# Attention in groups of two tiles: the order of one fused kernel changed

## The chip, the cores and the metric

The kernel runs on one core of a Trainium2 chip. A core has TensorE (matmuls), VectorE, ScalarE, GpSimd and SyncE, each with an instruction queue of its own; they meet only in semaphores. The metric is the device time of one execution in microseconds.

## What is computed

Three layers in a row, all in float32, for 2 batches of 768 positions and 512 channels:

```python
# 1. attention, 2 x 8 heads of 64: sinks (first 4 keys) and a window of 128 keys
keep = is_sink | ((rel >= 0) & (rel < window))
a = softmax(where(keep, q @ k.T / sqrt(64), -1e9));  x = a @ v      # heads side by side: [2, 768, 512]
# 2. mixing of positions
theta = x @ w_theta;  y = w_tok_r @ (x * cos(theta)) + w_tok_i @ (x * sin(theta))
u = x + y;  x = u + relu(u @ w_ch)
# 3. gated layer
h = relu(x @ w_in);  u, v = halves(h);  v = layer_norm(v)
out = (u * (w_spatial @ v + b_spatial)) @ w_out
```

The change touches attention and the first products with w_theta.

## The kernel before

A **pair** is two heads of one batch; there are eight pairs (n = 0..3, batch b = 0, 1, no = 2n + b), each of six **tiles** of 128 queries, 48 tiles m in all. A tile needs the keys of its own 128 positions, of the 128 before and of the sinks. Two heads stand in the two halves of the partitions.

What each engine does for tile m (i = m mod 6):

- **scores** (TensorE, L1079): six matmuls, three products of high and low parts for each head, and a bias of two small matmuls, into one of two banks s_ps. It waits until the exps of tile m-2 have read that bank.
- **maxima** (VectorE, L787): L793 folds the two key blocks into one, where the mask chooses, then one L799 for each head takes the maximum. Tile 0 of a pair needs no fold.
- **exps** (ScalarE, L521): one exp for each head, and its sum, into probs.
- **turn_probs** (TensorE, L1105): transposes of both heads' probabilities and, for i > 0, of the sinks', into pt_ps. **copy_pt** (ScalarE, L534) copies them to p_t; **diagonal** (VectorE, L802) multiplies them by the triangle into p_d.
- **times_v** (TensorE, L1119): 12 matmuls (4 for i = 0) of p_t and p_d with v_raw, v_sink and v_d into o_ps.
- After three tiles **copy_o** (ScalarE, L539) copies o_ps to x_raw, **turn_o** (TensorE, L1135) transposes it back into tr_ps, **normalise** (VectorE, L823) divides by the sums (**weights**, L814) into x_sb, **turn_x** (TensorE, L1142) transposes that, and **copy_x** (VectorE, L832) writes x_t.

The order is written out by hand in a function `pair` for each engine. TensorE's, for each tile: turn_probs(m), scores(m+2), times_v(m-1), and at four of six tiles a turn_o or turn_x. ScalarE's: copy_pt(m), exps(m+2), at two of six tiles copy_o. VectorE's: maxima(m+2), diagonal(m), at other tiles weights, normalise or copy_x. GpSimd meanwhile splits q and k of the next pair into high and low parts (`split_pair`), makes v_d (`v_steps`) and splits the token weights (`split_tok`); SyncE loads q, k, v and the token weights (L361 to L368).

After the last tile come the products with w_theta, `theta(t)` for 12 tiles t of 128 rows: x_high (ScalarE, L532) and x_low (VectorE, L811) split x_t into xth and xtl, TensorE does 12 matmuls, ScalarE and VectorE make sine and cosine of the result, `z_product` (L964) multiplies by x, and z_high (L633) and z_low (GpSimd, L468) split that for the token products (`token_block`). theta(0) and theta(1) stand around the last times_v. Then each engine meets a branch (L584, L878, L1204) to code for other masks, which isn't taken here; theta(2) to theta(11) stand behind it.

Of the kernel before, what the change touches and what calls it, by code (L numbers as in the profile page):

```python
# [6 lines left out]
F32 = mybir.dt.float32  # L7
# [18 lines left out]
HALVES = TILES // 2  # L26
TURNS = 2 * BATCH * KC
# [8 lines left out]
FOLD = P + SINKS  # L36
SCALE = 1.0 / math.sqrt(HD)
# [10 lines left out]
def attn_moe_gmlp(nc, q_t, k_t, v_p, v_s, n_sink, window, w_theta, w_tok, w_ch, w_in, w_sp, b_spatial, w_out, out):  # L48
    ctx = ExitStack()
    with ctx:  # L50
# [60 lines left out]
        x_raw = [at(f"x_raw{half}", o + 6144 + 16 * FOLD + 1536 * half, [P, HALVES, P], F32) for half in range(2)]  # L111
        probs = [at(f"probs{b}", o + 6144 + 8 * FOLD * b, [P, FOLD, 2], F32) for b in range(2)]
        o += 6144 + 16 * FOLD + 3072

        p_t = [at(f"p_t{b}", o + 1536 * b, [P, 3 * P], F32) for b in range(2)]
        p_d = [at(f"p_d{b}", o + 3072 + 1024 * b, [P, 2, P], F32) for b in range(2)]
# [14 lines left out]
        v_sink = [at(f"v_sink{b}", o + 512 * b, [P, P], F32) for b in range(2)]  # L131
        o += 1024
# [5 lines left out]
        q_hi = [at(f"q_hi{b}", o + 3072 * b, [P, SEQ], F32R) for b in range(2)]  # L138
        q_lo = [at(f"q_lo{b}", o + 6144 + 3072 * b, [P, SEQ], F32R) for b in range(2)]
        o += 12288  # L140
        k_hi = [at(f"k_hi{b}", o + 4 * K_COLS * b, [P, K_COLS], F32R) for b in range(2)]
        k_lo = [at("k_lo0", o + 8 * K_COLS, [P, K_COLS], F32R), k_lo_1]
        assert o + 12 * K_COLS <= xt_at
# [20 lines left out]
        xth = [at(f"xth{j}", e1_at + 4096 * j, [P, KC, P], F32R) for j in range(4)]  # L164
        xtl = [at(f"xtl{j}", e1_at + 4096 * j + 2048, [P, KC, P], F32R) for j in range(4)]
# [32 lines left out]
        den = at("den", small + 96, [P, HALVES, 2], F32)  # L198
        rden = at("rden", small + 128, [P, HALVES, 2], F32)
# [9 lines left out]
        pt_ps = [banks[2][:, b, :] for b in range(2)]  # L209
# [10 lines left out]
        s_clear = sem("pt_cleared")  # L220
# [6 lines left out]
        s_to = sem("o_turned")  # L227
        s_tr = sem("x_turned")
# [4 lines left out]
        s_ptc = sem("pt_copied")  # L233
        s_fold = sem("scores_folded")
# [107 lines left out]
        def _(sp):  # L342
# [1030 lines left out]
```

## Time and profile before

| what | value |
|---|---|
| median of 3 runs | 460.03 us (459.51 to 460.06) |
| the profiled execution | 460.16 us, its span 458.4 us |
| TensorE matmuls busy | 433.2 us (95%) |
| VectorE, ScalarE, GpSimd busy | 226.4, 168.9, 189.4 us |
| mean granted TensorE clock | 0.992 |

The span goes from the first to the last instruction. An engine's busy time counts its instructions, not its waits. Matmuls are pipelined, so their rows overlap: distances from start to start tell what one costs. In a row "x2" merges neighbours that are alike, and the time behind the start goes from the first one's start to the last one's end.

### The profile page before, as it was taken

The numbers are of one execution on the slowest core, as the hardware profiler recorded it, in microseconds if no ns is written. First come the engines' busy times: TensorE is split into PE (matmuls) and PEld (weight loads), VectorE is DVE, ScalarE is ACT, GpSimd is POOL, SyncE is SP. The second block draws the span as 40 slices with busy tenths as digits, with TensorE's granted clock in tenths as the row PEclk, the third lists the DMA queues.
The fourth block names the chain that finished last, engine by engine and source line by source line (L and its number), as shares of the span: only waits on it lengthen the run. The fifth ranks groups of instructions, "written<-read, shape, count | busy, mean of one in ns | idle before, by whom it ended". The sixth has DMA issues, their size and how long they took to land.

```text
span 458.4 us, 7198 instructions
## 1 busy us (share of the span) xinstructions
PE 433.2 (95%) x2712; PEld 369.9 (81%) x2712; DVE 226.4 (49%) x468; ACT 168.9 (37%) x418; POOL 189.4 (41%) x130
## 2 busy tenths in 40 slices
PE   0899999999986999999999999999999999999997
PEld 0577777777665879999999997887887889999885
DVE  4548777777736798333223555616515403332222
ACT  2336566566523875333224104524223311111221
POOL 3499778883000018886674400000000164433442
PEclk9999999999997999999999999999999999999999
DMA  3744533431000002001200014000002000000222
GB/s 124 268 146 157 173 124 137 158 117 42 1 1 6 1 0 93 0 1 65 119 0 2 0 42 200 1 0 1 0 0 92 0 1 1 0 0 0 86 99 92
DMA packets 9444, 26.94 MB, mean 59 GB/s; under 512 B 1217, under 2 KB 2241, under 8 KB 9409
## 3 DMA queue, kind: packets, MB, share of 16 engines
q1 hardware_dynamic: 7776, 21.24, 13.1%
q0 software_dynamic: 1344, 5.24, 3.2%
q8 instruction: 21, 0.34, 0.3%
q14 instruction: 15, 0.11, 0.1%
q10 hardware_dynamic: 288, 0.00, 0.0%
HBM read 23.33 MB, written 3.15 MB: 58 GB/s over the span
## 4 chain that ended last, share of the span: by engine, by line
PE 92%; DVE 3%; ACT 2%; issue 1%; DMA 1%; POOL 0%; SPq 0%; ACTq 0%; DVEq 0%
PE ps L1075 23%; PE ps L1077 22%; PE ps L1076 22%; PE ps L1132 8%; PE ps L1093 8%; PE ps L1111 3%; PE ps L1139 2%; PE ps L1145 2%; DMA k_raw<-in_k_t 1%; PE ps L1113 1%; DVE x2l L996 0%; DVE x L993 0%; PE ps L1100 0%; ACT x2h L691 0%; POOL zl L468 0%
## 5 line engine op out<-in xcount | busy, mean ns | idle before, releaser
L1075 PE MATMUL ps<-tok_hi,zl 128*128 128x384 f32 x192 | 64.2, 335 | 0.2 <-POOL zl L468 0.2
L1077 PE MATMUL ps<-tok_hi,zh 128*128 128x384 f32 x192 | 64.1, 334 | 0.0
L1076 PE MATMUL ps<-tok_lo,zh 128*128 128x384 f32 x192 | 64.1, 334 | 0.0
L526 ACT ACTIVATE probs<-ps,neg_max 128x160 f32<-128x160 f32 (+1 forms) x96 | 37.3, 401 | 46.6 <-DVE neg_max L799 46.4
L468 POOL TENSOR_TENSOR zl<-cos_sb,zh 128x768 fp32r<-128x768 f32 x8 | 18.9, 2365 | 65.4 <-ACT zh L633 65.3
L970 DVE TENSOR_TENSOR x_t<-ps,x_t 128x768 f32<-128x768 f32 x16 | 15.3, 957 | 58.9 <-PE ps L1077 58.9
L1075 PEld LDWEIGHTS ps<-tok_hi,zl 128*128 128x128 f32 x192 | 36.0, 188 | 0.6 <-POOL zl L468 0.6
L500 POOL DMA_DIRECT2D wo_raw<-in_moe_w_out x1 | 0.8, 785 | 86.1 <-PE ps L1077 86.1
L1076 PEld LDWEIGHTS ps<-tok_lo,zh 128*128 128x128 f32 x192 | 36.0, 188 | 0.0
L1077 PEld LDWEIGHTS ps<-tok_hi,zh 128*128 128x128 f32 x192 | 36.0, 188 | 0.0
L495 POOL TENSOR_TENSOR vl<-vn_sb,vh 128x768 fp32r<-128x768 f32 x8 | 19.6, 2446 | 37.2 <-ACT vh L683 37.2
L1075 PE MATMUL ps<-sp_hi,vl 128*128 128x384 f32 x96 | 32.2, 335 | 0.7 <-ACT gate_t L710 0.7
L1093 PE MATMUL ps<-k_hi,q_lo 64*128 64x288 f32 (+1 forms) x96 | 20.1, 414 | 13.3 <-DVE bias L780 13.3
L1076 PE MATMUL ps<-sp_lo,vh 128*128 128x384 f32 x96 | 32.1, 334 | 0.0
L1077 PE MATMUL ps<-sp_hi,vh 128*128 128x384 f32 x96 | 32.1, 334 | 0.0
L468 POOL TENSOR_TENSOR zl<-sin_sb,zh 128x768 fp32r<-128x768 f32 x8 | 20.8, 2602 | 20.6 <-ACT zh L633 20.6
L1053 DVE TENSOR_TENSOR mixed<-ps,b_row 128x768 f32<-128x768 f32 x8 | 7.7, 958 | 43.1 <-PE ps L1077 43.1
L799 DVE TENSOR_REDUCE neg_max<-ps 128x1 f32<-128x160 f32 (+1 forms) x96 | 26.1, 314 | 5.6 <-PE ps L1093 3.9
L1093 PEld LDWEIGHTS ps<-k_hi,q_lo 64*128 64x128 f32 x96 | 9.8, 201 | 22.8 <-issue 21.3
L793 DVE COPY_PREDICATED ps<-tri_r,ps 128x256 f32<-128x256 int32 x40 | 17.1, 429 | 21.3 <-PE ps L1093 21.3
L537 ACT ACTIVATE p_t<-ps 128x384 f32<-128x384 f32 (+1 forms) x48 | 22.8, 475 | 7.4 <-PE ps L1113 7.2
L515 POOL TENSOR_TENSOR gl<-gate_t,gh 128x512 fp32r<-128x512 f32 x12 | 15.4, 1283 | 22.8 <-ACT gh L732 22.8
(150 smaller groups left out, 1140.4 us busy)
## 6 DMA issues: line engine op xcount, KB each, us to landing
tok_raw<-in_w_tok SPq DMA_DIRECT2D x6, 768.0 KB, 7.5
k_raw<-in_k_t SPq DMA_DIRECT2D x8, 464.0 KB, 5.7
q_raw<-in_q_t SPq DMA_DIRECT2D x8, 384.0 KB, 4.2
v_raw<-in_v_p SPq DMA_DIRECT2D x8, 384.0 KB, 2.9
out<-o_sb SPq DMA_DIRECT2D x12, 256.0 KB, 2.0
sp_raw<-in_w_sp SPq DMA_DIRECT2D x3, 768.0 KB, 5.9
in_raw<-in_moe_w_in POOLq DMA_DIRECT2D x1, 2048.0 KB, 8.5
th_raw<-in_moe_w_theta POOLq DMA_DIRECT2D x1, 1024.0 KB, 5.7
```

Source lines behind the costliest of these rows:

```text
L468: pool.tensor_tensor(zl[turn % 2][:, :, :], trig[c][:, b * TILES:(b + 1) * TILES, n * P:(n + 1) * P], zh[turn % 2][:, :, :].bitcast(F32), ...
L495: pool.tensor_tensor(vl[b][:, :, :], vn_sb[:, b * TILES:(b + 1) * TILES, bass.ds(n * P, P)], vh[b][:, :, :].bitcast(F32), ALU.subtract).th ...
L515: pool.tensor_tensor(gl[b][:, :, :], gate_t[:, :, bass.ds((2 * n + b) * P, P)], gh[b][:, :, :].bitcast(F32), ALU.subtract).then_inc(s_gl[b ...
L526: act.activation(probs[i % 2][:, cols, h], s_ps[i % 2][:, h, cols], ACT.Exp, bias=neg_max[:, i % 2, h:h + 1], accum_out=sums[:, i, h:h + 1 ...
L537: act.activation(p_t[i % 2][:, cols], pt_ps[i % 2][:, cols], ACT.Copy).then_inc(s_ptc, 1)
L793: dve.copy_predicated(s_ps[i % 2][:, :, 0:P], tri_r[:, :].bitcast(I32).unsqueeze(1).broadcast_to([P, 2, P]), s_ps[i % 2][:, :, FOLD:FOLD + ...
L799: dve.tensor_reduce(neg_max[:, i % 2, h:h + 1], s_ps[i % 2][:, h, cols], AX.X, ALU.max, negate=True).then_inc(s_max, 1)
L1075: pe.matmul(dst, w_lo, m_hi, start=first, stop=False)
L1076: pe.matmul(dst, w_hi, m_lo, start=False, stop=False)
L1077: return pe.matmul(dst, w_hi, m_hi, start=False, stop=last)
L1093: mm = pe.matmul(s_ps[i % 2][:, h, 0:keys.stop - keys.start], q_part[rows, tile], k_part[rows, keys], start=(part == 0), stop=(part == 2))
L1132: mm = pe.matmul(o_ps[rows, cols], values[:, rows], turned[h], start=(j == 0), stop=(j == len(parts) - 1))
```

## The change

- A **group** g is two tiles, 2g and 2g+1; there are 24 (GROUPS). Each engine's order is now a loop over steps. TensorE in step s: scores(2s), scores(2s+1), times_v(s-2), turn_probs(s-1), turns(s-2). ScalarE: exps(2s), exps(2s+1), copy_pt(2s-2), copy_o(s-2), copy_pt(2s-1). VectorE: normalise(s-3), copy_x(s-4), maxima(2s), diagonal(2s-3), maxima(2s+1), weights(s-2), diagonal(2s-2).
- turn_probs(g) has five transposes: four of 128 probabilities and one for the sinks of both tiles. For that, probs is [128, 2, 160, 4]: the four (tile, head) values of a key lie side by side. v_sink gets a second half, so that either tile picks its rows.
- turns(g) is turn_o of group g and turn_x of group g-1 in one go, of two tiles each, in two halves of tr_ps. It waits for copy_o(g).
- maxima is one instruction for both heads; the denominators add a constant tile (eps) by tensor_tensor.
- theta(0) to theta(3) stand ahead of the branch, between the last groups' steps; xt_slot and theta_ps place them.
- split_tok goes ahead of v_steps on GpSimd. q, k and the slots of xth and xtl are placed otherwise.

```diff
 @block.scalar
+            def exps(m):
+                i = m % TILES
+                act.wait_ge(s_max, m + 1)
+                for h in range(2):
...
+                    act.activation(probs[:, m // 2 % 2, cols, 2 * (m % 2) + h], s_ps[i % 2][:, h, cols], ACT.Exp,
...
+            def copy_pt(m):
+                cols = slice(0, 2 * P if m % 2 else 3 * P)
+                act.wait_ge(s_pt, m // 2 + 1)
+                act.activation(p_t[:, m % 2, cols], pt_ps[:, m % 2, cols], ACT.Copy).then_inc(s_ptc, 1)
+            def copy_o(g):
+                act.wait_ge(s_pv, g + 1)
+                if g >= 2:
+                    act.wait_ge(s_turn, g - 1)
+                act.activation(x_raw[g % 2][:, :, :], o_ps[:, 0:2 * P].rearrange("p (t q) -> p t q", q=P),
                                ACT.Copy).then_inc(s_oc, 1)
+            for step in range(GROUPS):
+                exps(2 * step)
+                exps(2 * step + 1)
+                if step >= 1:
+                    copy_pt(2 * step - 2)
+                if step >= 2:
+                    copy_o(step - 2)
+                if step >= 1:
+                    copy_pt(2 * step - 1)
+            act.wait_ge(s_split, 5 * (2 * PAIRS - 1))
+            act.wait_ge(s_xt, GROUPS - HALVES - 2)
+            act.wait_ge(s_pv, GROUPS - HALVES)
+            for t in range(2):
                 x_high(t)
+            copy_o(GROUPS - 2)
+            for m in range(ALL_TILES - 2, ALL_TILES):
+                copy_pt(m)
+            act.wait_ge(s_xt, GROUPS - HALVES - 1)
+            for t in range(2, THETA_EARLY):
+                x_high(t)
+            copy_o(GROUPS - 1)
 @block.vector
-                for h in range(2):
-                    dve.wait_ge(s_sc, 2 * m + h + 1)
-                    dve.tensor_reduce(neg_max[:, i % 2, h:h + 1], s_ps[i % 2][:, h, cols], AX.X, ALU.max,
-                                      negate=True).then_inc(s_max, 1)
+                dve.wait_ge(s_sc, 2 * m + 2)
+                dve.tensor_reduce(neg_max[:, i % 2, :], s_ps[i % 2][:, :, cols], AX.X, ALU.max, negate=True).then_inc(s_max, 1)
+            for step in range(GROUPS + 2):
+                if step >= 3:
+                    normalise(step - 3)
+                if step >= 4:
+                    copy_x(step - 4)
+                if step < GROUPS:
+                    maxima(2 * step)
+                if 2 <= step:
+                    diagonal(2 * step - 3)
+                if step < GROUPS:
+                    maxima(2 * step + 1)
+                if step >= GROUPS:
+                    for t in range(2 * (step - GROUPS), 2 * (step - GROUPS) + 2):
+                        x_low(t)
+                if step >= 2:
+                    weights(step - 2)
+                if 1 <= step <= GROUPS and step % HALVES != 1:
+                    diagonal(2 * step - 2)
+            normalise(GROUPS - 1)
+            copy_x(GROUPS - 2)
+            copy_x(GROUPS - 1)
 @block.tensor
+            def turn_probs(g):
+                if g >= 1:
+                    no, _, _, i = place(2 * g - 1)
+                    pe.wait_ge(s_ptc, 2 * g)
+                    pe.wait_ge(s_ptd, diagonals(no, i))
...
+                for j in range(2):
+                    pe.wait_ge(s_exp, 4 * g + 2 * j + 2)
+                    for h in range(2):
+                        pe.transpose(pt_ps[:, j, h * P:(h + 1) * P], probs[:, g % 2, 0:P, 2 * j + h], ident[:, :])
+                pe.transpose(pt_ps[:, 0, WIN:WIN + P], probs[:, g % 2, P:FOLD, :].rearrange("p s j -> p (s j)"),
+                             ident[:, :]).then_inc(s_pt, 1)
+            def turns(g):
+                if g >= 1:
+                    pe.wait_ge(s_norm, g)
+                if g >= 2:
+                    pe.wait_ge(s_xt, g - 1)
+                if g < GROUPS:
+                    pe.wait_ge(s_oc, g + 1)
+                    for j in range(2):
+                        mm = pe.transpose(tr_ps[:, j * P:(j + 1) * P], x_raw[g % 2][:, j, :], ident[:, :])
+                if g >= 1:
+                    _, n, b, i = place(2 * (g - 1))
+                    for j in range(2):
+                        mm = pe.transpose(tr_ps[:, (2 + j) * P:(3 + j) * P], x_sb[:, b * TILES + i + j, n * P:(n + 1) * P],
+                                          ident[:, :])
+                mm.then_inc(s_turn, 1)
+            for step in range(GROUPS):
+                scores(2 * step)
+                scores(2 * step + 1)
+                if step >= 2:
+                    times_v(step - 2)
+                if step >= 1:
+                    turn_probs(step - 1)
+                if step >= 2:
+                    turns(step - 2)
+            times_v(GROUPS - 2)
+            turn_probs(GROUPS - 1)
+            turns(GROUPS - 2)
             pe.wait_ge(s_th_w, 2)
             theta(0)
+            times_v(GROUPS - 1)
             theta(1)
+            turns(GROUPS - 1)
+            pe.wait_ge(s_exp, 2 * ALL_TILES)
+            theta(2)
+            turns(GROUPS)
+            theta(3)
```

## Rows read from the trace of the kernel before

**Rows 1.** The page, chain that ended last: share of the span by engine.
```profile
PE 92%; DVE 3%; ACT 2%; issue 1%; DMA 1%; POOL 0%; SPq 0%; ACTq 0%; DVEq 0%
```

**Rows 2.** Stretches: from:to, length, busy us (instructions) of each engine, clock, DMA.
```profile
13.00:34.80 21.80, 21.48 (x132) 14.86 (x134) 9.62 (x32) 8.85 (x35) 17.02 (x11) 1.00 0.53 198
34.80:124.00 89.20, 87.71 (x934) 64.24 (x930) 68.48 (x199) 54.70 (x213) 61.15 (x47) 1.00 0.35 117
...
141.50:147.40 5.90, 5.84 (x14) 4.61 (x15) 4.09 (x8) 0.49 (x2) 0.00 (x0) 0.50 0.01 4
147.40:172.00 24.60, 24.41 (x109) 19.85 (x107) 22.08 (x42) 19.72 (x35) 1.85 (x1) 1.00 0.00 1
```

**Rows 3.** The chain in order of time: start us, us, what; one pair apart.
```profile
58.59 0.37 PE ps L1093 x4
...
72.06 0.37 PE ps L1093 x4
```

**Rows 4.** Timeline, 62.3 to 65.7 us: start us, us, instruction, idle before it.
```profile
62.42 0.41 DVE L805 TENSOR_TENSOR p_d<-ps,tri_c 128x256 f32<-128x256 f32 x1
...
62.75 0.55 DVE L834 COPY x_t<-ps 128x384 f32<-128x384 f32 x1
...
62.87 0.40 PE L1093 MATMUL ps<-k_hi,q_lo 64*128 64x288 f32 x2
...
63.06 0.38 ACT L537 ACTIVATE p_t<-ps 128x256 f32<-128x256 f32 x1
...
63.37 0.29 PE L1093 MATMUL ps<-k_hi,q_hi 64*128 64x288 f32 x2
...
63.59 0.44 PE L1132 MATMUL ps<-p_t,v_raw 128*64 128x128 f32 x4
63.73 0.43 DVE L793 COPY_PREDICATED ps<-tri_r,ps 128x256 f32<-128x256 int32 x1 [0.43 <-PE ps L1093]
...
63.85 0.39 PE L1132 MATMUL ps<-p_t,v_sink 128*64 128x128 f32 x4
...
64.07 0.39 PE L1132 MATMUL ps<-p_d,v_d 128*64 128x128 f32 x4
64.19 0.56 DVE L799 TENSOR_REDUCE neg_max<-ps 128x1 f32<-128x160 f32 x2
...
64.39 0.50 PE L1111 MATMUL ps<-ident,probs 128*128 128x128 f32 x2
...
64.55 0.41 ACT L526 ACTIVATE probs<-ps,neg_max 128x160 f32<-128x160 f32 x1 [1.11 <-DVE neg_max L799]
...
64.94 0.40 ACT L526 ACTIVATE probs<-ps,neg_max 128x160 f32<-128x160 f32 x1
64.94 0.40 PE L1093 MATMUL ps<-k_hi,q_lo 64*128 64x288 f32 x2
...
65.31 0.49 ACT L543 ACTIVATE x_raw<-ps 128x384 f32<-128x384 f32 x1
...
65.68 0.50 ACT L537 ACTIVATE p_t<-ps 128x384 f32<-128x384 f32 x1
```

**Rows 5.** Groups by line and shape, 42 to 104 us: xcount | busy, mean ns.
```profile
L799 DVE TENSOR_REDUCE neg_max<-ps 128x1 f32<-128x160 f32 x45 | 12.5, 319 | 0.8
```

**Rows 6.** End of attention: timelines, and the branch lines' own instructions (ns, start).
```profile
123.83 0.29 PE L1093 MATMUL ps<-k_hi,q_hi 64*128 64x288 f32 x2
...
L1204 PEldq COMPARE_BRANCH  x1: 3437/3437/3437, 137.9 to 137.9; - x1
...
L878 DVEq TENSOR_LOAD <-general x1: 549/549/549, 139.7 to 139.7; - x1
...
143.31 1.29 DVE L811 TENSOR_TENSOR xtl<-x_t,xth 128x512 fp32r<-128x512 f32 x2 [2.88 <-issue]
...
150.73 0.69 DVE L811 TENSOR_TENSOR xtl<-x_t,xth 128x512 fp32r<-128x512 f32 x1 [1.79 <-ACT xth L532]
...
171.97 0.44 PE L1075 MATMUL ps<-tok_hi,zl 128*128 128x384 f32 x1 [0.19 <-POOL zl L468]
```

More of the change, by code:

```diff
@@ L36 @@
 FOLD = P + SINKS
+THETA_EARLY = 4
 SCALE = 1.0 / math.sqrt(HD)
@@ L110, in attn_moe_gmlp @@
         v_raw = [at(f"v_raw{b}", o + 3072 * b, [P, TILES, P], F32) for b in range(2)]
[L111 to L116, printed above, removed]
+        x_raw = [at(f"x_raw{g}", o + 6144 + 1024 * g, [P, 2, P], F32) for g in range(2)]
+        probs = at("probs", o + 8192, [P, 2, FOLD, 4], F32)
+        o += 8192 + 4 * 8 * FOLD
+        p_t = at("p_t", o, [P, 2, 3 * P], F32)
+        p_d = at("p_d", o + 3072, [P, 2, 2, P], F32)
         v_d = [at(f"v_d{b}", o + 5120 + 2560 * b, [P, TILES - 1, P], F32) for b in range(2)]
@@ L129, in attn_moe_gmlp @@
         o += 768
-        v_sink = [at(f"v_sink{b}", o + 512 * b, [P, P], F32) for b in range(2)]
-        o += 1024
+        v_sink = [at(f"v_sink{b}", o + 1024 * b, [P, 2, P], F32) for b in range(2)]
+        o += 2048
         k_lo_1 = at("k_lo1", o, [P, K_COLS], F32R)
@@ L208, in attn_moe_gmlp @@
         s_ps = banks[0:2]
-        pt_ps = [banks[2][:, b, :] for b in range(2)]
+        pt_ps = banks[2]
         o_ps = banks[3][:, 0, :]
@@ L862, in _, with weights @@
[L862 to L875 removed]
+            def weights(g):
+                i = 2 * g % TILES
+                dve.wait_ge(s_exp, 4 * g + 4)
+                dve.tensor_tensor(den[:, :, :], sums[:, i:i + 2, :], eps[:, :, :], ALU.add).then_inc(s_den, 1)
+                dve.wait_ge(s_den, 2 * g + 1)
+                dve.reciprocal(rden[:, :, :], den[:, :, :]).then_inc(s_den, 1)
@@ new lines, in normalise @@
+            def normalise(g):
+                _, n, b, i = place(2 * g)
+                dve.wait_ge(s_den, 2 * g + 2)
+                dve.wait_ge(s_turn, g + 1)
+                rows = slice(b * TILES + i, b * TILES + i + 2)
+                dve.tensor_tensor(x_sb[:, rows, n * P:(n + 1) * P].rearrange("p t (h d) -> p t h d", h=2),
+                                  tr_ps[:, 0:2 * P].rearrange("p (t h d) -> p t h d", t=2, h=2),
+                                  rden[:, :, :].unsqueeze(3).broadcast_to([P, 2, 2, HD]), ALU.mult).then_inc(s_norm, 1)
@@ L1077, in product, with scores @@
                 return pe.matmul(dst, w_hi, m_hi, start=False, stop=last)
[L1079 to L1081 removed]
+            def scores(m):
+                pair_no, _, b, i = place(m)
+                if pair_no == 0:
                     pe.wait_ge(s_first, 4)
@@ new lines, in times_v @@
+                    if t:
+                        for h in range(2):
+                            rows = slice(h * HD, (h + 1) * HD)
+                            pe.matmul(o_ps[rows, cols], v_sink[b][:, j, rows], p_t[:, 0, WIN:WIN + P], start=False, stop=False)
+                        pe.wait_ge(s_ptd, diagonals(no, t))
+                        for h in range(2):
+                            rows = slice(h * HD, (h + 1) * HD)
+                            mm = pe.matmul(o_ps[rows, cols], v_d[b][:, t - 1, rows], p_d[:, j, h, :], start=False, stop=True)
@@ L1251, in token_block @@
                     pe.wait_ge(s_u, turn - 1)
+                if turn == 1:
+                    for half in range(2):
+                        pe.wait_ge(s_theta_used[half], 5)
                 pe.wait_ge(s_zl, turn + 1)
```

285 lines of the change are left out of this document (76 added, 209 removed).

## Prediction

> **What bounds the kernel now.** I read the page first, then the kernel by stretches, the chain in order of time, the timeline of one tile and the rows around the attention's end. The page gives TensorE 92% of the chain that ended last [rows 1]. The stretches show that this holds in attention too: from 34.8 to 124 us TensorE is busy 87.7 of 89.2 us, VectorE 68.5, ScalarE 54.7 [rows 2]. Before 34.8 us the same matmuls go at the lower level: 132 in 21.8 us (6.1 per us) against 934 in 89.2 us (10.5 per us), though that row's granted clock reads 1.00 [rows 2]. The chain shows the rhythm: one pair of heads (six tiles) takes 72.06 - 58.59 = 13.47 us, 4.49 us for two tiles, and every piece of it is TensorE's [rows 3].
>
> So the others matter only where they make TensorE wait. The reader should see in [rows 4] how long their own chain is: the last scores matmul starts at 63.37 and the fold (L793) at 63.73, 0.36 later; fold to maximum 0.46 (63.73 to 64.19); maximum to exp 0.36 (64.19 to 64.55, its own 0.32 and 0.04 across); exp to exp 0.39, exp to copy 0.37, copy of 384 columns to the next 0.37 (64.55, 64.94, 65.31, 65.68); a diagonal of 0.41 lets VectorE's next start after 0.33 (62.42 to 62.75). Today half of this chain lies beside each tile's V and turning.
>
> **TensorE's own work in the new order.** Start to start [rows 4]: scores of a tile 63.59 - 62.87 = 0.72; V 64.39 - 63.59 = 0.80, of which four matmuls inside take 0.22 (63.85 to 64.07) and the last four 0.32 (64.07 to 64.39), so the switch to another kind costs 0.10; turning of three 64.94 - 64.39 = 0.55, where again the first is 0.1 dearer and the last 0.1. A group of two is then: scores 2 x 0.72 = 1.43; V 1.46 with one switch fewer; five transposes instead of six 0.68; four turnings 4 x 0.11 and the switch 0.53. Sum 4.10 us. A group with tile 0 has about 0.5 less (4 V matmuls for 12, shorter scores), so a pair needs 3 x 4.10 - 0.5 = 11.8 us against 13.47. That is the gain on offer, 1.7 us a pair.
>
> One rule speaks to this term. The Trainium skill, TensorEngine Tiling (Array Packing), Key Properties, says that changing the tiling mode drains the TensorE, tiles of one mode not. The rows agree (0.10 at each switch), and by that rule alone the attention would gain the 1.7 us a pair: way (1) below.
>
> **What the order adds: a wait in every group.** Step s on TensorE is: scores of both tiles, V of group s-2, transposes of group s-1, turns of group s-2. The turns wait for copy_o(s-2). On ScalarE copy_o(s-2) stands behind exps(2s), exps(2s+1) and copy_pt(2s-2); and copy_pt(2s-2) waits for the transposes that TensorE finished just before. So TensorE cannot pass from transposes to turns before two ScalarE copies have run: end of the last transpose 0.27 with 0.04 to ScalarE, copy_pt of 384 columns 0.37 to the next start, copy_o of 256 columns 0.38 (the row of that width) and 0.07 back, less the 0.11 the transpose would have taken anyway: 1.0 us [rows 4]. (The 0.27 is a transpose's start to end: 0.50 for two spaced 0.22.) TensorE's round is then 4.10 + 1.0 = 5.1 us.
>
> A second round of the same length goes through VectorE. From the first turn: four turns 0.33, the switch 0.20, scores 0.50 to the last pair, 0.36 to the fold = 1.39 (VectorE's normalise and copy_x, 0.33 each, fit beside it: 0.64 + 0.66 = 1.30). Then fold 0.46, maximum 0.40, diagonal 0.33, fold 0.46, maximum to exp 0.52, two exps 0.76, copy_pt 0.37, copy_o 0.45. Sum 5.14 us. The merged maximum is in no row: it lies between one instruction's 0.32 [rows 5] and the two's 0.56 [rows 4]. The copies of 256 and 384 columns (0.38, 0.50) show 0.9 ns a column, so 160 columns more give 0.32 + 0.15, rounded to 0.48, and the next start 0.08 before its end as behind the diagonal, 0.40. Normalise and copy_x of 256 columns are taken as the diagonal, of that width too: 0.33. Nothing is left to hide the wait: queued behind the turns are the next scores, which VectorE and then ScalarE need, and normalise and copy_x stand ahead of the next maxima.
>
> I take 5.14 us, and 4.9 where tile 0 has no fold: 15.2 to 15.3 us a pair, 2.55 us a tile, against 13.47 and 2.245. Bounds: without the second round and with half the wait 4.6 a group (break-even is 4.49), with all latencies 5% longer 5.4.
>
> **Sum for attention.** Today 40 tiles go from 34.8 to the last scores at 123.83 [rows 6]. In the slow first part the matmuls go at 10.5 / 6.1 = 1.7 times the time, so two tiles take 4.49 x 1.7 = 7.6 us at most (less, where the wait for another engine doesn't stretch; 7.2 taken); the new order has that less 0.4 and the wait of 1.0, 7.7 to 7.9. But its first steps have no V and no turns, which puts it some 3 us ahead after eight tiles; at 34.8 us it stands near tile 8.1 where before stands at 7.4. Then 39 tiles x 2.55 = 99.4, so the last scores end at 134.2: +10.4 us (2.50 to 2.65 a tile: +8.5 to +14).
>
> **End of attention.** What starts token mixing is not TensorE's theta products but the sine and cosine work: the first token matmul at 171.97 waits for zl, 28.66 us after VectorE's first subtraction behind its branch, 143.31 [rows 6]. Before: last scores to 143.31 is 19.5 us. After, from the last scores: 3.1 until turns(21) (0.5 to their fold, then 0.46, 0.52, 0.76, 0.37, 0.45 as above), then turns 0.55, V 1.46, transposes 0.7, turns 0.55, theta(0) 2.7, V 1.46, theta(1) 2.7, turns 0.55, theta(2) 2.7, last turns 0.35, to copy_x 0.3 = 17.1 (a product is 12 matmuls at 24.41 / 109 [rows 2]). VectorE's branch comes after: from its load at 139.7 to 143.31 is 3.6 us [rows 6]; 20.7 in all, 1.2 later than before. In return all theta products are there when asked for: VectorE's gaps, the largest 1.79 before 150.73 [rows 6], 2.4 in total, go, and ScalarE reaches the first z some 0.9 earlier. Net: -2.1 us. TensorE's branch, 3437 ns [rows 6], now runs beside theta(3) (2.7) and leaves about 1.7 us idle instead of 3.7; the slow matmuls that followed it (granted clock 0.50 from 141.5 to 147.4 [rows 2]) should go. That frees TensorE 4 us earlier, but it then waits for zl, so it is no further gain; its end is the bound of this term (-4.6), and no gain at all (0) the other.
>
> **Edits at no cost.** VectorE's denominators (tensor_tensor instead of L818), the eps and probs memsets, v_sink of twice the size (its DMA lands beside 10 us of other work), split_tok ahead of v_steps (GpSimd needs some 10.8 us a pair of now 15) and the waits for s_theta_used: all lie beside TensorE's 5.1 us rounds; without cover each is under 0.5 us.
>
> **Total.** 460.16 + 10.4 - 2.1 = 468.5. The rhythm of before adds up from such rows some 2% too short (13.2 for 13.47); 2% of 99.4 is 2.0, and I take half, as the copies' latencies were read directly: +1.0. Forecast 469.5. The profiled execution (460.16, span 458.4) is 0.13 above the median of 460.03, so no correction.
>
> **Other ways.** (1) Faster: copy_o is ready in time and TensorE stays the bound: 39 tiles x 1.96 = 76 us, the last scores at 111, 13 earlier, and 2.1 at the end: 445. For it: TensorE's 98% now. Against: copy_o's place behind copy_pt in ScalarE's order, which no duration moves; it decides when the wait falls below 0.4 us a group. (2) The wider spacing of probs costs. Each probability now lies four words from the next instead of two. The transposes read it and the exps write it. At two words the transposes of probs take (0.55 - 0.2) / 3 = 0.12 each beside the V matmuls' 0.11 for a couple [rows 4]; no row has four words. Bounds: nothing, or one more element time per element (0.11 a transpose, 0.1 an exp): 0.4 to 0.6 a group over 20 groups, 8 to 12 us more: 480. The Trainium skill, Advanced Engine Details and Errata, SBUF Cachelines, says that a line is 16 bytes and two hits on it are needed for full speed; at four words there is one hit. By that rule this case is the outcome; no trace here shows it. (3) TensorE, idle a fifth of the time, loses its clock for a while: at the lower level a group takes 7.8 instead of 5.14, so a third of the stage at it costs 17 us: 487. Against it: only an idle of 3.7 us has brought the clock down so far [rows 2, 6]. (4) The wait is half as long: 4.6 a group, 461.
>
> **Chances.** Forecast 0.64 (464 to 476), (1) 0.10, (2) 0.16, (3) 0.06, (4) 0.04. Leaving out (1) and most of (3), the range is 461 to 483. Faster by over 0.2% (about what a measurement of this kernel can tell from none) 0.12, within 0.02, slower 0.86.
>
> **What would show it.** In the new profile: a group of two at 5.1 us; before each group's turns TensorE idle for 0.9 to 1.1 us with x_raw as releaser; TensorE about 80% busy from 35 to 134 us; the first token matmul near 180 to 181; transposes of probs spaced 0.12. The forecast is wrong if that idle is under 0.4 us, if exps or transposes grew, or if the matmuls show the lower level after 40 us.

## The result, and the profile after

| | kernel before | kernel after | ratio (95% interval) |
|---|---|---|---|
| first comparison, median | 459.77 us (457.29 to 460.06, 4 runs) | 482.62 us (478.30 to 484.48, 4 runs) | 1.052 (1.046 to 1.057) |
| second comparison (e10 below), median | 459.75 us (455.89 to 460.94, 7 runs) | 477.74 us (476.27 to 482.46, 4 runs) | 1.040 (1.034 to 1.046) |

The change costs 5% and 4%. The forecast, 469.5, had the sign and the waits that the order makes, but not the falls of the granted clock; it was 13 us too low in the first comparison and 8 in the second. The profiled execution of the first is the fastest of its four: 478.30 us, span 476.1, mean granted clock 0.975; the others have 0.964 to 0.972.

The chain of the page answers to [rows 1]: TensorE is down from 92% to 78% of it, VectorE and ScalarE are up from 3 and 2.

```profile
PE 78%; DVE 10%; ACT 7%; issue 3%; DMA 1%; POOL 0%; SPq 0%; ACTq 0%
```

The same stage by stretches (columns as in [rows 2]). TensorE was busy 98% of the time and is now busy 77% of 42 to 59.8 us and 75% of 107.5 to 131.3. Between them lies a stretch of a kind that the kernel before has nowhere in attention: at a granted clock of 0.50 TensorE issues 91 matmuls in 13.5 us, 6.7 per us, against 8.6 and 8.2 beside it. There are four such falls, of 3.4, 3.4, 13.7 and 3.4 us, 23.9 us in all, beginning at 59.8, 76.8, 93.9 and 131.4.

```profile
42.00:59.80 17.80, 13.76 (x153) 10.60 (x153) 12.84 (x32) 9.09 (x36) 15.66 (x13) 1.00 0.60 207
94.00:107.50 13.50, 12.55 (x91) 10.03 (x90) 6.70 (x18) 4.72 (x19) 8.12 (x6) 0.50 0.02 6
107.50:131.30 23.80, 17.96 (x195) 13.49 (x195) 14.01 (x40) 12.23 (x47) 10.24 (x8) 1.00 0.25 81
```

One step in the timeline, from turns to turns (answers to [rows 4]).

```profile
65.19 0.41 PE L1145 MATMUL ps<-ident,x_raw 128*128 128x128 f32 x2 [0.95 <-ACT x_raw L560]
...
65.93 0.43 DVE L836 TENSOR_TENSOR x_sb<-ps,rden 128x256 f32<-128x256 f32 x1 [0.69 <-PE ps L1149]
...
66.27 0.41 DVE L843 COPY x_t<-ps 128x256 f32<-128x256 f32 x1
...
66.61 0.43 DVE L804 COPY_PREDICATED ps<-tri_r,ps 128x256 f32<-128x256 int32 x1
...
67.07 0.49 DVE L809 TENSOR_REDUCE neg_max<-ps 128x2 f32<-128x320 f32 x1
...
67.47 0.41 DVE L814 TENSOR_TENSOR p_d<-ps,tri_c 128x256 f32<-128x256 f32 x1
...
67.81 0.42 DVE L804 COPY_PREDICATED ps<-tri_r,ps 128x256 f32<-128x256 int32 x1
...
68.26 0.49 DVE L809 TENSOR_REDUCE neg_max<-ps 128x2 f32<-128x320 f32 x1
...
68.67 0.15 DVE L827 TENSOR_TENSOR den<-sums,eps 128x4 f32<-128x4 f32 x1
68.78 0.55 ACT L541 ACTIVATE probs<-ps,neg_max 128x160 f32<-128x160 f32 x1 [0.24 <-DVE neg_max L809]
...
69.03 0.27 PE L1108 MATMUL ps<-ident,probs 128*128 128x128 f32 x1
...
69.19 0.54 ACT L541 ACTIVATE probs<-ps,neg_max 128x160 f32<-128x160 f32 x1
...
69.57 0.49 ACT L553 ACTIVATE p_t<-ps 128x384 f32<-128x384 f32 x1
...
69.94 0.40 ACT L560 ACTIVATE x_raw<-ps 128x256 f32<-128x256 f32 x1
...
70.48 0.41 PE L1145 MATMUL ps<-ident,x_raw 128*128 128x128 f32 x2 [1.18 <-ACT x_raw L560]
```

From 65.19 to 70.48 is 5.29 us for two tiles. The last transpose starts at 69.03 and the turns at 70.48; between them TensorE has nothing it may do. VectorE's instructions from 66.61 to 68.26 follow each other without idle time, then come the exps and the two copies: the second round that the forecast followed. It is the one that decides here. The transposes end at 69.30, but copy_pt starts only at 69.57, straight behind the second exp.

TensorE's waits from 20 to 142 us (total, times, longest), and the merged maximum among the groups of 42 to 104 us (answers to [rows 5]):

```profile
PE ps L1145 <- ACT x_raw L560: 22.1, 20, 1.3
```

```profile
L809 DVE TENSOR_REDUCE neg_max<-ps 128x2 f32<-128x320 f32 x17 | 8.3, 491 | 0.6
```

The attention's end in the timeline (answers to [rows 6]): last scores matmul, VectorE's first subtraction behind it, TensorE's first product behind its own, first token matmul.

```profile
143.82 0.29 PE L1084 MATMUL ps<-k_hi,q_hi 64*128 64x288 f32 x2
...
165.19 1.29 DVE L820 TENSOR_TENSOR xtl<-x_t,xth 128x512 fp32r<-128x512 f32 x2 [3.01 <-ACT xth L547]
...
166.03 0.47 PE L1066 MATMUL ps<-th_hi,xtl 128*128 128x512 f32 x1 [1.56 <-DVE xtl L820]
...
189.80 0.44 PE L1066 MATMUL ps<-tok_hi,zl 128*128 128x384 f32 x1 [1.77 <-POOL zl L483]
```

The last scores are 20.0 us later than before (143.82 against 123.83), and the stretch from there to the first token matmul is 2.2 us shorter (45.98 against 48.14). From that matmul on both kernels take the same: 286.3 of 476.1 and 286.4 of 458.4 us.

### The profile page after: what moved, and what is told of

Its sections match the earlier page's. It is cut to its first block, busy times and chain, and to the rows that moved or that the text cites. A ratio compares the mean times of both kernels' runs of the same rounds, so it can differ in the third digit from the quotient of the medians.

```text
span 476.1 us, 7064 instructions
## 1 busy us (share of the span) xinstructions
PE 428.6 (90%) x2696; PEld 372.1 (78%) x2696; DVE 226.0 (47%) x453; ACT 170.1 (36%) x426; POOL 190.0 (40%) x130
## 3 DMA queue, kind: packets, MB, share of 16 engines
q0 software_dynamic: 1344, 5.24, 3.1%
## 4 chain that ended last, share of the span: by engine, by line
PE 78%; DVE 10%; ACT 7%; issue 3%; DMA 1%; POOL 0%; SPq 0%; ACTq 0%
PE ps L1066 20%; PE ps L1067 20%; PE ps L1068 20%; PE ps L1084 7%; ACT probs L541 2%; PE ps L1145 2%; PE ps L1124 2%; PE ps L1107 2%; DVE neg_max L809 2%; ACT x_raw L560 1%; PE ps L1129 1%; PE ps L1133 1%; DMA k_raw<-in_k_t 1%; ACT p_t L553 1%; PE ps L1149 1%
## 5 line engine op out<-in xcount | busy, mean ns | idle before, releaser
L541 ACT ACTIVATE probs<-ps,neg_max 128x160 f32<-128x160 f32 (+1 forms) x96 | 44.7, 540 | 64.1 <-DVE neg_max L809 64.1
L961 DVE TENSOR_TENSOR x_t<-ps,x_t 128x768 f32<-128x768 f32 x16 | 15.3, 957 | 58.6 <-PE ps L1068 58.5
L1145 PE MATMUL ps<-ident,x_raw 128*128 128x128 f32 x48 | 10.0, 292 | 24.6 <-ACT x_raw L560 24.6
L1084 PE MATMUL ps<-k_hi,q_lo 64*128 64x288 f32 (+1 forms) x96 | 18.7, 386 | 14.5 <-DVE bias L790 13.7
L1145 PEld LDWEIGHTS ps<-ident,x_raw 128*128 128x128 f32 x48 | 5.0, 143 | 29.5 <-issue 28.3
L1084 PEld LDWEIGHTS ps<-k_hi,q_lo 64*128 64x128 f32 x96 | 10.4, 211 | 19.1 <-issue 18.9
L814 DVE TENSOR_TENSOR p_d<-ps,tri_c 128x256 f32<-128x256 f32 x40 | 16.7, 419 | 18.0 <-ACT p_t L553 18.0
L809 DVE TENSOR_REDUCE neg_max<-ps 128x2 f32<-128x320 f32 (+1 forms) x48 | 23.0, 480 | 4.2 <-PE ps L1084 2.7
```

Source lines behind the costliest of these rows:

```text
L541: act.activation(probs[:, m // 2 % 2, cols, 2 * (m % 2) + h], s_ps[i % 2][:, h, cols], ACT.Exp, bias=neg_max[:, i % 2, h:h + 1], accum_out ...
L809: dve.tensor_reduce(neg_max[:, i % 2, :], s_ps[i % 2][:, :, cols], AX.X, ALU.max, negate=True).then_inc(s_max, 1)
L814: dve.tensor_tensor(p_d[:, m % 2, :, :], pt_ps[:, m % 2, 0:2 * P].rearrange("p (h q) -> p h q", h=2), tri_c[:, :].unsqueeze(1).broadcast_t ...
L961: dve.tensor_tensor(x_t[part].rearrange("p o (h t) -> p (o h) t", h=2), banks[turn % 2][:, :, 0:HALFSEQ], x_t[part].rearrange("p o (h t) - ...
L1084: mm = pe.matmul(s_ps[i % 2][:, h, 0:keys.stop - keys.start], q_part[rows, tile], k_part[rows, keys], start=(part == 0), stop=(part == 2))
L1145: mm = pe.transpose(tr_ps[:, j * P:(j + 1) * P], x_raw[g % 2][:, j, :], ident[:, :])
```

## The experiments

Theory A was the forecast's: the wait for copy_o and the round through VectorE make the loss. What the forecast left unexplained was some 13 us, so theory C: TensorE's many short waits bring the granted clock down. Rivals: the four-word spacing of the probabilities costs (B, D), and the falls belong to one chip.

All times are medians; the kernel before ran beside each of them on the same chip.

| run | after, with | us | before beside it | ratio (95%) | clock of the runs |
|---|---|---|---|---|---|
| e10 | nothing changed | 477.74 | 459.75 | 1.040 (1.034 to 1.046) | 0.964 to 0.982 |
| e1 | copy_o first | 459.93 | 457.15 | 1.005 (1.002 to 1.009) | 0.993 to 1.000 |
| e2 | probabilities two words apart | 472.13 | 457.15 | 1.034 (1.027 to 1.041) | 0.995 to 1.000 |
| e3 | 8 idle transposes in the wait | 468.89 | 457.15 | 1.025 (1.019 to 1.031) | 0.996 to 1.000 |
| e7 | 2 of them | 467.04 | 457.90 | 1.019 (1.014 to 1.024) | 0.995 to 1.000 |
| e12 | 2 of them, beside e10 | 467.32 | 459.75 | 1.019 (1.014 to 1.025) | 0.996 to 1.000 |
| e11 | 1 of them, beside e10 | 467.30 | 459.75 | 1.018 (1.013 to 1.024) | 1.000 |
| e4b | turns a step later, TensorE only | 471.08 | 457.90 | 1.027 (1.022 to 1.031) | 0.985 to 0.989 |
| e4 | the same and VectorE's order | 447.61 | 457.15 | 0.980 (0.974 to 0.986) | 0.992 to 1.000 |
| e455 | e4, copy_o first, two words | 452.62 | 457.90 | 0.984 (0.977 to 0.991) | 0.988 to 0.999 |
| e9 | e4, theta(2), (3) behind the branch | 452.63 | 457.58 | 0.989 (0.983 to 0.994) | 0.984 to 0.989 |
| e8 | e4, w_theta split last | 444.45 | 457.58 | 0.973 (0.967 to 0.978) | 0.988 to 1.000 |
| e8c | e8, copy_o first | 443.63 | 457.58 | 0.969 (0.964 to 0.975) | 0.996 to 1.000 |
| e6 | the kernel *before*, four words | 458.66 | 457.90 | 1.000 (0.996 to 1.004) | 0.991 to 0.996 |

**e1: copy_o ahead of both copies of p_t.**

```diff
+                if step >= 2:
+                    copy_o(step - 2)
                 if step >= 1:
                     copy_pt(2 * step - 2)
-                if step >= 2:
-                    copy_o(step - 2)
```

> The changed kernel with one exchange on ScalarE: in each step copy_o(s-2) goes ahead of copy_pt(2s-2). In the changed kernel a group takes 5.29 us at the full clock, and 9.9 us more were lost to spells at the lower level. Theory A (the turns wait for copy_o, which stands behind exps and copy_pt): TensorE's own round loses the wait (5.2 to about 4.1) and VectorE's round loses the 0.37 us of copy_pt, so the latter decides, 4.7 to 4.9 us a group, 0.4 to 0.5 less over 23 groups: 9 to 12 us faster than the changed kernel (466 to 472), and a few us more if TensorE, less idle, keeps its clock. Theory B (the probabilities' spacing makes exps and transposes dear, the order is harmless): the exchange changes nothing, 478 to 484.

Measured 459.93 us, 18 to 23 us below the kernel after; the expectation was too small. The timeline: copy_o now runs straight behind the exps, copy_pt (here merged with the next one) behind it, and the turns start 4.91, 4.91 and 4.51 us apart.

```profile
66.76 0.41 PE L1145 MATMUL ps<-ident,x_raw 128*128 128x128 f32 x2 [0.79 <-ACT x_raw L560]
...
71.14 0.39 ACT L560 ACTIVATE x_raw<-ps 128x256 f32<-128x256 f32 x1
...
71.40 0.78 ACT L553 ACTIVATE p_t<-ps 128x384 f32<-128x384 f32 x2
...
71.67 0.41 PE L1145 MATMUL ps<-ident,x_raw 128*128 128x128 f32 x2 [0.94 <-ACT x_raw L560]
...
76.18 0.41 PE L1145 MATMUL ps<-ident,x_raw 128*128 128x128 f32 x2 [0.21 <-ACT x_raw L560]
```

A pair has three groups: 14.33 us against 15.83 (5.29, 5.29, 5.25), 1.50 x 7 pairs = 10.5 us. The other 7 to 12 us are the falls, of which one of 3.4 us is left (at 43.4, right behind waits of 0.93 us at 40.4 and, for q_lo, 1.07 at 42.1). Moving one copy in ScalarE's order, the place that the forecast named as the cause, takes nearly all the loss away.

**e2: probabilities two words apart.**

```diff
-        probs = at("probs", o + 8192, [P, 2, FOLD, 4], F32)
+        probs = at("probs", o + 8192, [P, 2, 2, FOLD, 2], F32)
...
-                pe.transpose(pt_ps[:, 0, WIN:WIN + P], probs[:, g % 2, P:FOLD, :]...
+                for j in range(2):
+                    mm = pe.matmul(pt_ps[j * 2 * SINKS:(j + 1) * 2 * SINKS, 0, WIN:WIN + P], ...
```

> The changed kernel with the probabilities two words apart, as before the change, instead of four; the sinks of the two tiles are then turned by two identity matmuls into the two halves of the partitions instead of one transpose, and v_sink's rows lie in that order. Theory B (the spacing costs): exps last 0.40 us instead of 0.54, two of them on each group's chain, so 0.3 us less a group and 6 to 8 us less in all (471 to 475). Theory A: the exps are shorter in the profile too, but from one exp's start to the next there were 0.40 us already against 0.387 before, so a group gains 0.05 us at most, and the two matmuls take that back: 0 to 1 us, same as the changed kernel within the scatter that its clock makes.

Measured 472.13. On the time alone this would have gone to B. The trace says otherwise: the exps are back at 0.40 us, but the groups are no shorter (5.25, 5.51 and 5.34, 16.1 us a pair against 15.83; the layout needs two small matmuls instead of one transpose). What is gone are the falls: one of 3.4 us in the profiled run instead of four, 23.9 us together, and two of the four runs have a mean clock of 1.000. The two matmuls are TensorE's extra work in each group, which points to C.

**e6: the kernel before, four words apart**, the same question without the new order.

```diff
-                    act.activation(probs[i % 2][:, cols, h], s_ps[i % 2][:, h, cols], ACT.Exp,
+                    act.activation(probs[i % 2][:, cols, h, 0], s_ps[i % 2][:, h, cols], ACT.Exp,
```

> The kernel before with each probability four words from the next instead of two, nothing else. The exps should be recorded at 0.54 us instead of 0.40, as in the kernel after, but start 0.39 us apart as before, and the transposes keep 0.12 us. Theory: same time within 0.5%, clock about 0.99. Rival (the spacing costs 0.4 to 0.6 us a group of two, or brings down the clock by itself): 466 to 475 us.

Ratio 1.000 (0.996 to 1.004), with the clock of the kernel before. B and D are out, for the order of before; for the new order D is answered by e7, e11 and e12, which keep four words. The group of the exps shows what the spacing does: 46 of them at 550 ns, where the kernel before has 0.41 and 0.40 [rows 4].

```profile
L526 ACT ACTIVATE probs<-ps,neg_max 128x160 f32<-128x160 f32 x46 | 21.7, 550 | 20.7 <-DVE neg_max L799 20.7
```

An exp lasts 0.15 us longer, but in the kernel after the next one starts 0.40 us behind it (68.78, 69.19), against 0.39 before [rows 4].

**e3: eight transposes of the identity in the wait**, work that nobody needs.

```diff
+                if 2 <= g < GROUPS - 2:
+                    for _ in range(8):
+                        pe.transpose(tr_ps[:, 2 * P:3 * P], ident[:, :], ident[:, :])
```

> The changed kernel with eight transposes of the identity (0.88 us at the full clock) put where TensorE waits for copy_o in groups 2 to 21, into the half of tr_ps that the turns overwrite: work that nothing needs. Theory C (TensorE's clock falls in attention because TensorE is idle a fifth to a quarter of the time): the spells at the lower level go or become rarer, the groups stay at 5.3 us at the full clock since the filler fits into a wait of 1.3 us, and the kernel is 5 to 10 us faster than the changed one (470 to 476). If the clock falls for another reason, the spells stay (20 to 30 us of them) and the kernel is not faster, or slower by up to 5 us, as the filler takes 1.7 us at the lower level.

Measured 468.89, 1 us under the expected range: more work, and 9 to 14 us less time. The groups take 5.23, 5.24 and 5.18 us. In the profiled run the clock rises at 34.1 us and doesn't fall before 160.4, behind the theta products; there it falls for 3.4 us.

**e7, e12, e11: two transposes, two again, one.**

> The kernel after, with 2 transposes of the identity instead of 8 ahead of each group's turns, where TensorE waits 1.3 us for copy_o. They are 0.22 us of work a group and lie in the wait, so the round should stay 5.29 us. Theory C (TensorE's idle time alone makes the granted clock fall): the wait left is some 1.1 us, about what the kernel with probabilities two words apart has (1.0 us a group, one fall of 3.4 us, 472.1 us), so the falls get few: 469 to 475 us. Rival D (the four-word spacing of the probabilities, not the idle time, is what makes the clock fall, and 8 transposes merely outweighed it): the falls stay, 478 to 484 us.

> The kernel with two transposes of the identity in each wait, on the same chip as the kernel after. Theory: 466 to 469 us, clock above 0.99, 12 to 17 us below the kernel after. Rival (chip): no more than 3 us below the kernel after.

> The kernel after with one transpose of the identity, 0.11 us of work, ahead of each group's turns. Two of them took every fall away (467.0 us). Theory (the kernel after stands just beyond the edge of what keeps the clock): between the two, 467 to 478 us, at least one run without a fall in attention. Rival (the two fillers helped by another way, by making the turns' first matmul cheap, 0.07 us a group, 1.4 us in all): 477 to 483 us.

e7 measured 467.04, e12 467.32, e11 467.30: all have the clock as C has it. e7 came out 2 us under its expected range and e11 at the low end of its own. e12 is within its range too, but only 10.4 us below the kernel after (e10, 477.74) and not 12 to 17. One transpose is as good as two. Eight falls in the two profiles of the kernel after; none in attention in these three.

**e10: the kernel after again, on the chip of e11 and e12.**

> The kernel after, unchanged, beside two neighbours of it on one chip: its falls of the granted clock (mean 0.964 to 0.975) were seen on one chip only, and the kernels without falls ran on others. Theory (the falls belong to the kernel: TensorE idle 1.3 us in each group): 478 to 485 us, clock 0.96 to 0.98, falls between 40 and 145 us. Rival (they belong to that chip or that hour): 467 to 471 us with a clock above 0.99.

Measured 477.74, 0.3 us under the expected range, with falls in all four runs. The profiled run (482.46) has falls of 13.7, 3.4, 3.4 and 13.7 us. The same two stretches in it and in e11, first e10, then e11:

```profile
42.00:57.40 15.40, 13.54 (x96) 10.83 (x97) 7.74 (x21) 5.78 (x24) 13.17 (x11) 0.56 0.30 109
57.40:81.00 23.60, 17.75 (x194) 13.27 (x192) 14.94 (x40) 12.23 (x47) 13.11 (x11) 1.00 0.55 185
```

```profile
42.00:57.40 15.40, 12.74 (x142) 9.79 (x142) 12.13 (x30) 8.16 (x34) 13.52 (x12) 1.00 0.53 175
57.40:81.00 23.60, 19.26 (x216) 14.91 (x218) 16.21 (x42) 12.26 (x49) 18.54 (x15) 1.00 0.41 143
```

In the first 15.4 us e10 does 96 matmuls where e11 does 142. The fall belongs to the kernel, not to a chip, and one matmul of 0.11 us in each wait decides it. It also takes two semaphore waits off the turns (last section): the idle time left is 0.75, 0.98 and 1.11 us in the three groups of a pair instead of 0.95, 1.18 and 1.31, and a group is 0.06 us shorter. Whether the work done or the shorter idle time keeps the clock isn't separated by this. The price in one fall: the groups around a 3.4 us fall take 6.83 instead of 5.29 (1.54 more), those in a 13.7 us fall 7.89 and 7.93 (5.2 more). That makes 9.9 us in the first profile and 13.6 in e10's.

**e4: the turns a step later, and VectorE's maxima first.**

```diff
                 scores(2 * step + 1)
+                if step >= 3:
+                    turns(step - 3)
                 if step >= 2:
                     times_v(step - 2)
...
-                if step >= 2:
-                    turns(step - 2)
+            turns(GROUPS - 3)
@@ VectorE: normalise(step - 3) and copy_x(step - 4) from ahead of maxima(2 * step) to behind maxima(2 * step + 1)
```

> The changed kernel with the turns of a group one step later: TensorE does scores, scores, turns(s-3), V(s-2), transposes(s-1); VectorE does normalise(s-3) and copy_x(s-4) behind both maxima instead of ahead. Nothing waits any more for a copy made in the same step. Theory A: both rounds of 5.2 us are gone and TensorE's own work is the bound, 4.0 to 4.2 us a group: 25 us less at the full clock, and the lower level's 9.9 us mostly too: 444 to 452 us, faster than the kernel before (460). Theory B (costs of spacing, memory or more instructions, not order): no more than a few us less, 474 to 482.

Measured 447.61, faster than before by 2.0% (1.4 to 2.6). TensorE's 47 to 110 us, three groups, and the one long wait:

```profile
47.00:110.00 63.00, 63.00 (x732) 49.99 (x734) 56.81 (x145) 44.21 (x171) 50.89 (x39) 1.00 0.42 140
```

```profile
41.73 0.33 PE L1084 MATMUL ps<-k_hi,q_lo 64*128 64x128 f32 x2 [3.57 <-POOL q_lo L442]
...
60.82 0.44 PE L1145 MATMUL ps<-ident,x_raw 128*128 128x128 f32 x2
...
64.90 0.44 PE L1145 MATMUL ps<-ident,x_raw 128*128 128x128 f32 x2
...
68.72 0.44 PE L1145 MATMUL ps<-ident,x_raw 128*128 128x128 f32 x2
...
72.80 0.44 PE L1145 MATMUL ps<-ident,x_raw 128*128 128x128 f32 x2
```

The fall of 3.4 us that is left begins at 43.3, behind that long wait. From 47 us on TensorE is busy 63.00 of 63.00 us, and a pair takes 4.08 + 3.82 + 4.08 = 11.98 us: TensorE's own work, forecast as 11.8. The last scores start at 112.6, where rival (1) of the prediction put them at 111.

**e4b: the first half of e4 alone**, VectorE's order left as it was.

> The kernel after with the turns of group s-3 behind the scores of step s on TensorE, as in the faster kernel, but VectorE's order left alone: normalise and copy_x stand ahead of the maxima. Theory (there are two rounds of about equal length, one from transposes over two ScalarE copies to the turns, one from the turns over normalise and copy_x into the maxima and exps): taking away the first alone gives little, a group 5.1 to 5.2 us, 462 to 470 us if the clock stays, up to 480 if it falls. Rival (only TensorE's wait for copy_o matters): 444 to 452 us.

Measured 471.08, just above the expected range and far from the rival: a pair takes 5.41 + 5.42 + 4.90 = 15.73 us, no less than after's 15.83. TensorE's wait has moved from x_raw to p_d:

```profile
PE ps L1133 <- DVE p_d L814: 7.7, 8, 1.3
```

(from 50 to 104 us). So the late turns alone gain nothing as long as normalise and copy_x stand ahead of the maxima. The round that bounds e4b is not quite the second round of the forecast, though: with the turns behind the scores it goes from turns (58.90) over normalise, copy_x, maximum and diagonal (59.66, 60.00, 60.33, 60.66) to V's product with p_d (61.13), the transposes (61.50), the scores (62.29) and the next turns (63.80). VectorE's half of e4 by itself was not run. The clock fell here too, three times for 3.4 us in the profiled run (at 73.8, 90.9 and 138.7), though the long wait is now for p_d and stands in another place.

**e455: e4 with copy_o first and two words.**

> The faster kernel (turns one step later on TensorE, normalise and copy_x behind the maxima on VectorE) with copy_o ahead of both copies of p_t on ScalarE and with probabilities two words apart. Theory: TensorE is the bound there, a group at 4.08 us, so neither matters: 446 to 450 us, the two extra small matmuls a group costing up to 0.25 us x 23 = 5 us more: up to 453. Rival (the exps' longer time or ScalarE's order still sets a part): 440 to 445 us.

Measured 452.62. A pair takes 4.33 + 4.33 + 4.08 = 12.74, 0.76 more than e4's: the two small matmuls, 0.25 a group, as the theory has it. 7 x 0.76 = 5.3 us: the four-word layout of the change, which needs one transpose in their place, is worth 5 us once TensorE is the bound.

**e9: theta(2) and theta(3) behind the branch again.**

```diff
-            theta(2)
             turns(GROUPS)
-            theta(3)
...
-            for t in range(THETA_EARLY, GT):
+            for t in range(2, GT):
```

> The faster kernel (447.6 us) with theta(2) and theta(3) behind TensorE's branch, as before the change; the splits of x_t for them stay ahead of it. Theory (the early products spare VectorE its waits behind its branch, 2.4 us, and ScalarE 0.9 us, and keep TensorE's idle time at its branch short): last scores to first token matmul 47.5 to 49.5 us instead of 45.7, the granted clock falls behind the branch as it does in the kernel before, 449.5 to 452 us. Rival (the early products are hidden anyway, the 2.2 us came from something else): 446.5 to 448.5 us.

Last scores to first token matmul: 48.97 us against e4's 45.73, within the expected 47.5 to 49.5. TensorE's idle time at its branch and the fall behind it are back, as in the kernel before [rows 2, 6]:

```profile
135.12 0.70 PE L1066 MATMUL ps<-th_hi,xtl 128*128 128x512 f32 x1 [3.64 <-issue]
```

```profile
135.00:138.60 3.60, 3.48 (x8) 2.76 (x9) 3.60 (x7) 0.00 (x0) 0.00 (x0) 0.53 0.02 7
```

The total of 452.63 is 0.6 above what was expected and not that difference alone: the profiled run also had a fall of 10.2 us at 39.6, where e4 has one of 3.4.

**e8 and e8c: what e4's own long wait was.** GpSimd's q_lo of the third pair came at 41.7, because the splitting of w_theta (6.5 us) stands ahead of it.

```diff
             v_steps(1, 1)
             split_tok(0)
-            pool.wait_ge(s_th_raw, 16)
...
             v_steps(2 * PAIRS - 1, 1)
+            pool.wait_ge(s_th_raw, 16)
...
```

> The faster kernel (turns one step later, normalise and copy_x behind the maxima) with GpSimd's splitting of w_theta (6.5 us of its time, in two instructions) moved from behind the second pair to behind the last one. In the faster kernel TensorE waits 3.6 us once, at 38 us, for q_lo of the third pair, which stands behind that splitting, and the granted clock is 0.5 for 3.4 us right after it. Theory: wait and fall go, 3.6 + about 1.6 us: 441 to 444 us. Rival (the splitting then delays the first theta product or the loads of the last pairs, or the clock falls elsewhere): 446 to 450 us.

> The same with copy_o ahead of both copies of p_t on ScalarE. Theory (with the turns a step later TensorE never waits for copy_o): within 1 us of the kernel without it. Rival (p_t's first copy comes later by 0.38 us and TensorE's V waits for it): 2 to 8 us slower.

e8 measured 444.45 (443.55 to 449.65), 0.5 above the expected range: wait and fall are gone in the profiled run (the run of 449.65 has a mean clock of 0.988), but one late group takes 5.93 us instead of 4.08. The cause is in the last section. e8c, 443.63, is the best kernel of the study: 3.1% faster than before (2.5 to 3.6%), and with the turns late the place of copy_o no longer matters.

## Why the prediction was right or wrong

**TensorE's own work (4.10 a group, 11.8 a pair): right.** e4 measures 4.08 and 11.98.

**The wait that the order adds (1.0): right where it decides.** In the third of the groups whose scores hold a tile 0, copy_pt waits for the transposes and TensorE is idle for 0.95 us, at L1145 with x_raw as releaser, as said. In the other two thirds it is idle for 1.18 and 1.31, because there the second round decides. e1 shows that both depend on the order on ScalarE.

**The second round (5.14, and 4.9 with tile 0): right in kind, 0.15 and 0.35 short.** 5.29 and 5.25. Its terms hold one by one (first turn to fold 1.42, fold 0.46, maximum 0.40, diagonal 0.34, fold 0.45, maximum to exp 0.52, exps 0.79, copy_pt 0.37). Off is copy_o to turns, 0.54 instead of 0.45. The first term holds by VectorE's own queue: normalise came 0.74 behind the turns, not 0.64, and the fold stood straight behind copy_x. And I let tile 0 shorten the second round without asking whether the first one, 5.1 by my own sum, then decides; it did. A pair is 15.83 and not 15.2 to 15.3. Over 39 tiles that is 3.5 us. It was made up for by the beginning: the clock rose at 25.6 us and not at 34.8. Without its falls the kernel would have ended its scores at 143.8 - 9.9 = 133.9, which leaves 37.6 tiles of 2.64 us from 34.8 on and not 39. That the forecast says 134.2 is luck: two errors of 3.5 to 4 us against each other.

**Sum without the falls: right, with that luck in it.** e11, which has one more transpose and no fall, takes 467.3 us. Its groups are 0.18 us a pair shorter (5.23, 5.23, 5.19), so the kernel after without falls would be at 467.3 + 7 x 0.18 = 468.6. Forecast 469.5.

**The granted clock: the step that failed.** The change cost 22.9 us in the first comparison where 9.5 had been forecast, and the difference is, to within 1 us, the term that the sum put at nothing: the loss of the clock. I gave rival (3) a chance of 0.06 and left it out of the sum because "only an idle of 3.7 us has brought the clock down so far". The trace of before could not carry that: in attention its TensorE is busy 98% of the time, so it holds no row of a TensorE that waits a little in every group. I had forecast just that, a wait of 1.0 in 5.1 us, and took the nearest row for the whole rule. The price in that rival (a group 7.8 us at the lower level, a third of the stage, 17 us) was about right: 7.89 and 7.93 measured for the two groups that hold a fall of 13.7 us, the low stretches 23.9 of 100 us in one profile and 34 in the other. What the falls cost is 9.9 us in the first profiled run, and by the medians 482.6 - 468.6 = 14 us in the first comparison and 9 in the second. e11 shows it on one chip: with the falls gone, 10.4 us less.

The Trainium skill, TensorE: Matmul & The Clock Gate, "HAM oscillation — how this bites in real kernels", warns of long waits between bursts; the section behind it, "A second HAM failure mode: psum-queue depth-cycling", tells of a kernel whose TensorE idles briefly between groups of matmuls and whose clock goes up and down. The trace agrees with the second in what the clock does, though the waits here are for a ScalarE copy (from 20 to 142 us none is over 1.31 us, and there are four falls), and my prediction did not weigh it. One chance for (3) as an amount added to the forecast, not as another outcome, would have been the better form: forecast and (3) happened together.

**The spacing of the probabilities, way (2), chance 0.16: did not come.** e6 shows no loss. The rule on SBUF Cachelines (the Trainium skill, Advanced Engine Details and Errata) shows in the exps' length, 0.55 against 0.41 us, not in the time between their starts, nor in the transposes (0.12 apart in both).

**End of attention (-2.1): right, by two misses that cancel.** -2.2 measured, and e9 gives 3.2 back. Last scores to VectorE's first subtraction behind its branch took 21.4 us (forecast 20.7), from there to the first token matmul 24.6 (forecast 25.4). VectorE stood still for 3.44 us at its branch (161.75 to 165.19), forecast 3.6; the row names ScalarE's xth, but the one that this subtraction needs was written by 162.89. TensorE waits 1.56 instead of 3.72 and its clock stays up there.

**Edits at no cost: right for the kernel after**, with one hidden price that e8 laid open (next section but one).

## What to carry to other kernels

When a change makes the fullest engine wait a little in every step, ask two things beyond the length of the wait: what else has a round of the same length (here the round through VectorE: with TensorE's turns a step later and VectorE's order left, a pair took 15.73 instead of 15.83 us, with both changed 11.98), and whether that engine's clock survives the pattern. A wait behind another engine's copy is a matter of order: one step more of distance between producer and consumer turned a loss of 4 to 5% into a gain of 2%, with the same work. Where a clock fall is suspected, put an instruction that nobody needs into the wait. It is the cheapest test, and here it gave back what the falls cost (10.4 us on one chip), though not the wait itself: e11 is still 1.8% slower than the kernel before.

## What the runs showed of the hardware

**A clock that falls under short waits.** In the kernel after TensorE waits 0.95, 1.18 and 1.31 us in the three groups of a pair, once in each 5.29 us. Both profiled runs lost the granted clock four times in about 100 us, to 0.50, for 3.4 or 13.7 us at a time, and all eight runs have a mean clock of 0.964 to 0.982. The twelve runs with one or two more transposes in each wait have 0.995 or more. All eight profiled falls begin 0.7 to 1.4 us behind the end of a wait of 1.31 us, the longest kind; four of the twelve such waits from 42 us on passed without one. The first of them, its wait and the stretch of its fall:

```profile
58.37 0.41 PE L1145 MATMUL ps<-ident,x_raw 128*128 128x128 f32 x2 [1.31 <-ACT x_raw L560]
```

```profile
59.80:63.20 3.40, 3.40 (x34) 3.00 (x31) 3.07 (x6) 1.81 (x8) 3.40 (x3) 0.50 0.14 55
```

But no length sorts all runs. e4b (0.87, 1.30 and 0.34 us) fell three times, e2 (0.95 to 1.02 in every group) once, and e11 (up to 1.11) never; e1 (0.21 to 0.94 in 4.8 us) keeps its clock but for one fall early on. What decides between them is open.

**VectorE held by GpSimd.** In e8 the sum of two small tiles, which takes 0.15 us alone (68.67 above), took 3.63 us, and ended 0.01 us after GpSimd's subtraction of w_theta (a row of each in the timeline; GpSimd's lengths are rough):

```profile
101.26 4.55 POOL L472 TENSOR_TENSOR th_lo<-th_raw,th_hi 128x2048 fp32r<-128x2048 f32 x1
...
102.19 3.63 DVE L827 TENSOR_TENSOR den<-sums,eps 128x4 f32<-128x4 f32 x1
```

All behind it on VectorE waited, and TensorE for its diagonal: the group of 5.93 us. In the kernel after ten such sums lasted 0.5 to 1.6 us and fell into VectorE's own waits. VectorE's instructions that read PSUM kept their lengths beside the same GpSimd work (normalise at 101.53 and copy_x at 101.86: 0.41 us each). The Trainium skill, SBUF — State Buffer, "Who interferes with whom", has the rule (a VectorE instruction with both inputs in SBUF and a GpSimd one that reads SBUF share a port pair as a lock, and the second to come waits); the trace agrees, and it decides where a long GpSimd instruction may stand.

**A wait less on the turns.** With one idle transpose ahead, copy_o's start to the turns' is 0.44 us (68.05 to 68.49 in e11) instead of 0.54. In the kernel after the turns' first matmul carries three waits, in e11 only the last. That these waits are the reason is argued, not shown.
